# Whole weights loaded and rounded on GpSimd for the third and fourth products, in a fused attention and two-layer kernel

## The reference

```python
scores = scale * np.matmul(q, k.transpose(0, 1, 3, 2))      # 4 batches, 12 heads, 448 tokens, head size 64
scores = cap * np.tanh(scores / cap)
attn = softmax(scores)                                      # the sum plus 1e-09
x = np.matmul(attn, v)                                      # put together to 1792 x 768
gate = 1.0 / (1.0 + np.exp(-(x @ w_gate)))                  # 768 x 1536
z = (gate * (x @ w_val)) @ w_out                            # 1536 x 768
h = z @ w_in                                                # 768 x 2048
y = (h * np.cos(h)) @ w_out2                                # 2048 x 768
```

## Time and profile before

| | us |
|---|---|
| median of 3 runs | 1211.96 (1211.85 to 1212.06) |
| the profiled execution | 1210.31 |
| its span, first to last instruction | 1208.3 |
| TensorE busy | 1197.2 (99%) |
| VectorE, ScalarE, GpSimd busy | 634.4, 558.5, 516.1 |
| moved by DMA | 293.95 MB, of it 58.98 MB written to HBM |

### The profile page before, as it was taken

The page is one execution under the profiler, slowest core; times in us unless marked ns, Lnnn a source line. Parts: engine busy times, 40 slices in busy tenths (PEclk is TensorE's granted clock), DMA queues, the critical chain, the costliest instruction groups (busy, mean ns, idle before and its releaser), DMA issues.

```text
span 1208.3 us, 16807 instructions
## 1 busy us (share of the span) xinstructions
PE 1197.2 (99%) x5932; PEld 1090.2 (90%) x5932; DVE 634.4 (53%) x1227; ACT 558.5 (46%) x1053; POOL 516.1 (43%) x458
## 2 busy tenths in 40 slices
PE   7999999999999999999999999999999999999998
PEld 5779999999999999999999999999999999999998
DVE  8951158876763477776651255877662211105610
ACT  8941155656541467766650257766662011105610
POOL 7969968879653356661113416663302000000000
PEclk9999999999999999999999999999999999999999
DMA  4579986799777678787668668887768566666663
GB/s 160 163 244 324 321 304 232 244 324 322 294 269 253 216 249 247 241 259 263 244 223 278 237 202 269 252 246 243 252 226 265 194 225 211 216 220 217 240 232 108
DMA packets 137746, 293.95 MB, mean 243 GB/s; under 512 B 48192, under 2 KB 57152, under 8 KB 137664
## 3 DMA queue, kind: packets, MB, share of 16 engines
q1 hardware_dynamic: 134064, 287.37, 70.7%
q10 hardware_dynamic: 3600, 5.51, 1.2%
HBM read 219.39 MB, written 58.98 MB: 230 GB/s over the span
## 4 chain that ended last, share of the span: by engine, by line
PE 95%; ACT 2%; DVE 2%; issue 1%; DMA 0%; SPq 0%; ACTq 0%
PE acc L846 27%; PE acc L847 27%; PE acc L845 27%; PE s_ps L743 3%; PE s_ps L744 3%; PE acc L798 2%; PE t_ps L815 2%; PE t_ps L817 1%; PE t_ps L780 1%; PE t_ps L764 1%; PE acc L835 1%; PE acc L837 1%; ACT prob L1030 1%; ACT h_lo_whole L1045 0%; DMA qk_in_whole<-qk 0%
## 5 line engine op out<-in xcount | busy, mean ns | idle before, releaser
L845 PE MATMUL acc<-h_hi,w_hi 128*128 128x448 f32 x672 | 247.8, 369 | 0.0
L846 PE MATMUL acc<-h_lo,w_hi 128*128 128x448 f32 x672 | 246.0, 366 | 0.0
L847 PE MATMUL acc<-h_hi,w_lo 128*128 128x448 f32 x672 | 245.7, 366 | 0.0
L845 PE MATMUL acc<-x_hi,w_hi 128*128 128x448 f32 x576 | 211.3, 367 | 0.0
L846 PE MATMUL acc<-x_lo,w_hi 128*128 128x448 f32 x576 | 210.9, 366 | 0.0
L847 PE MATMUL acc<-x_hi,w_lo 128*128 128x448 f32 x576 | 210.8, 366 | 0.0
L566 POOL TENSOR_TENSOR pt_lo<-pt_lo_whole,pt_hi 128x1344 fp32r<-128x1344 f32 x24 | 75.0, 3126 | 218.5 <-ACT pt_hi L1074 218.5
L847 PE MATMUL acc<-z_hi,w_lo 128*128 128x448 f32 x384 | 140.4, 366 | 0.0
L845 PE MATMUL acc<-z_hi,w_hi 128*128 128x448 f32 x384 | 140.4, 366 | 0.0
L846 PE MATMUL acc<-z_lo,w_hi 128*128 128x448 f32 x384 | 140.4, 366 | 0.0
L847 PEld LDWEIGHTS acc<-h_hi,w_lo 128*128 128x128 f32 x672 | 126.4, 188 | 10.0
(11 more groups left out here) (142 smaller groups left out, 2052.0 us busy)
## 6 DMA issues: line engine op xcount, KB each, us to landing
w_lo<-w_pair SPq DMA_DIRECT2D x156, 384.0 KB, 3.9
w_hi<-w_pair SPq DMA_DIRECT2D x156, 384.0 KB, 3.2
w_lo_whole<-w SPq DMA_DIRECT2D x52, 384.0 KB, 4.0
w_pair<-w_lo SPq DMA_DIRECT2D x52, 384.0 KB, 4.7
w_pair<-w_hi SPq DMA_DIRECT2D x52, 384.0 KB, 5.1
w_lo<-w_pair SPq DMA_DIRECT2D x36, 512.0 KB, 4.3
w_hi<-w_pair SPq DMA_DIRECT2D x36, 512.0 KB, 3.6
qk_in_whole<-qk SPq DMA_DIRECT2D x35, 512.0 KB, 6.2
```

The source lines that it names most:

```text
L845: e.matmul(out[:, 0:S], w_hi[u % HI][:, wb, :], a_hi[:, kb, :], start=first, stop=False)
L846: e.matmul(out[:, 0:S], w_hi[u % HI][:, wb, :], a_lo[:, kb, :], start=False, stop=False)
L847: return e.matmul(out[:, 0:S], w_lo[u % LO][:, wb, :], a_hi[:, kb, :], start=False, stop=last)
```

## The change

The high parts of the third and fourth products' weights are no longer stored. In batches 1 to 3 their whole weights are loaded from the inputs into the w_hi tiles, and GpSimd rounds them where they lie, in an instruction that stands one half ahead in the third product and two ahead in the fourth. TensorE waits for that rounding in place of the load. The waits of the other units are written anew. GpSimd's work for one attention pair in the third product stands at other places.

```diff
+KEPT_UNITS = FIRST[3]
+ROUNDED_AHEAD = {3: 1, 4: 2}
...
-    w_hi = [sb(f"w_hi{p}", [P, 2 * HALF_MAX, P], F32R) for p in range(HI)]
+    w_hi, w_hi_whole = zip(*[sb_both(f"w_hi{p}", [P, 2 * HALF_MAX, P]) for p in range(HI)])
...
-    kept = {s: nc.dram_tensor(f"w{s}_pair", (UNITS_OF[s], 2, 2, P, BLK[s], P), F32, kind="Internal").ap()
+    kept = {s: nc.dram_tensor(f"w{s}_pair", (UNITS_OF[s], 2, 1 + (FIRST[s] < KEPT_UNITS), P, BLK[s], P), F32, kind="Internal").ap()
...
+    def rounded_in_place(b, u, h):
+
+        return 2 * ((b - 1) * (UNITS - KEPT_UNITS) + u - KEPT_UNITS) + h + 1
+
+    def high_loaded(b, u):
+
+        return 16 * ((u + (b - 1) * UNITS) // HI + 1)
...
-                e.dma_start(kept[stage][j, h, 1, :, :, :], f32(w_lo[u % LO])[:, part, :]).then_inc(s_lokept[u % LO][h], 16)
-                e.dma_start(kept[stage][j, h, 0, :, :, :], f32(w_hi[u % HI])[:, part, :]).then_inc(s_hikept[u % HI][h], 16)
+                e.dma_start(kept[stage][j, h, 0, :, :, :], f32(w_lo[u % LO])[:, part, :]).then_inc(s_lokept[u % LO][h], 16)
+                if u < KEPT_UNITS:
+                    e.dma_start(kept[stage][j, h, 1, :, :, :], f32(w_hi[u % HI])[:, part, :]).then_inc(s_hikept[u % HI][h], 16)
...
                 e.wait_ge(s_acc, 2 * (u - HI) + h + 1)
-                e.dma_start(f32(w_hi[u % HI])[:, part, :], kept[stage][j, h, 0, :, :, :]).then_inc(s_hild[u % HI][h], 16)
+                if unit_no(stage, j) < KEPT_UNITS:
+                    e.dma_start(f32(w_hi[u % HI])[:, part, :], kept[stage][j, h, 1, :, :, :]).then_inc(s_hild[u % HI][h], 16)
+                else:
+                    w = {3: w3, 4: w4}[stage]
+                    e.dma_start(w_hi_whole[u % HI][:, part, :], w[j, h, :, :, :]).then_inc(s_hild[u % HI][h], 16)
...
+            def round_w(b, stage, j, h):
+
+                u, part = unit_no(stage, j), slice(h * HALF_MAX, h * HALF_MAX + BLK[stage])
+                e.wait_ge(s_hild[u % HI][h], high_loaded(b, u))
+                rounded(w_hi[u % HI][:, part, :], w_hi_whole[u % HI][:, part, :]).then_inc(s_round, 1)
+
+            def round_ahead(b, n):
+
+                for stage in ROUNDED_AHEAD:
+                    m = n + ROUNDED_AHEAD[stage]
+                    if m < len(halves) and halves[m][0] == stage:
+                        round_w(b, *halves[m])
...
-                if stage == 3 and 2 * j + h in (3, 5):
-                    moved_low(first + FOURTH // NG, j - 1)
-                if stage == 3 and 2 * j + h == 4:
+                if stage == 3 and 2 * j + h in (5, 8):
+                    moved_low(first + FOURTH // NG, (j - 2) // 2)
+                if stage == 3 and 2 * j + h == 6:
                     split_v(first + FOURTH // NG, 1)
...
-                    n, u = u + (b - 1) * UNITS, u + b * UNITS
-                    e.wait_ge(s_hild[u % HI][h], 16 * (n // HI + 1))
-                    e.wait_ge(s_lold[u % LO][h], 16 * (n // LO + 1))
+                    if u < KEPT_UNITS:
+                        e.wait_ge(s_hild[u % HI][h], high_loaded(b, u))
+                    else:
+                        e.wait_ge(s_round, rounded_in_place(b, u, h))
+                    e.wait_ge(s_lold[u % LO][h], 16 * ((u + (b - 1) * UNITS) // LO + 1))
```

More of the change, by code:

```diff
@@ L174, in build @@
     s_wld = [[sem(f"w_whole_loaded{p}{h}") for h in range(2)] for p in range(LO)]
-    s_whi, s_wsplit = sem("w_hi_done"), sem("w_split")
+    s_whi, s_wsplit, s_round = sem("w_hi_done"), sem("w_split"), sem("w_hi_rounded_in_place")
     s_hikept = [[sem(f"w_hi_kept{p}{h}") for h in range(2)] for p in range(HI)]
@@ L381, in unit_no @@
         return FIRST[stage] + j
+    halves = [(stage, j, h) for stage in (1, 2, 3, 4) for j in range(UNITS_OF[stage]) for h in range(2)]
+    def rounded_in_place(b, u, h):
+        return 2 * ((b - 1) * (UNITS - KEPT_UNITS) + u - KEPT_UNITS) + h + 1
+    def high_loaded(b, u):
+        return 16 * ((u + (b - 1) * UNITS) // HI + 1)
     block = nc.Block()
@@ L433, in all_kept @@
                     for p in range(HI):
-                        e.wait_ge(s_hikept[p][h], 16 * len(range(p, UNITS, HI)))
+                        e.wait_ge(s_hikept[p][h], 16 * len(range(p, KEPT_UNITS, HI)))
                     for p in range(LO):
@@ L440, in load_low @@
                 e.wait_ge(s_acc, 2 * (u - LO) + h + 1)
-                e.dma_start(f32(w_lo[u % LO])[:, part, :], kept[stage][j, h, 1, :, :, :]).then_inc(s_lold[u % LO][h], 16)
+                e.dma_start(f32(w_lo[u % LO])[:, part, :], kept[stage][j, h, 0, :, :, :]).then_inc(s_lold[u % LO][h], 16)
             def load_high(b, stage, j, h):
@@ L505, in behind @@
                     move_other_blocks(pair_of(b, i + 1), r // 2)
-            halves = [(stage, j, h) for stage in (1, 2, 3, 4) for j in range(UNITS_OF[stage]) for h in range(2)]
             def just_done(b, n):
@@ L624, in split_w @@
                     e.wait_ge(s_acc, 2 * (u - HI) + h + 1)
-                    e.wait_ge(s_hikept[u % HI][h], 16 * (u // HI))
+                    e.wait_ge(s_hikept[u % HI][h], 16 * (min(u, KEPT_UNITS) // HI))
                 rounded(hi, whole).then_inc(s_whi, 1)
@@ L711, in _ @@
             for b in range(B):
[L712 to L720, removed]
+                for n, (stage, j, h) in enumerate(halves):
+                    if b == 0 and (stage, j, h) not in early:
+                        split_w(stage, j, h)
+                    if b == 0:
+                        split_heads(b, stage, j, h)
+                    if b > 0:
+                        round_ahead(b, n)
+                    if b > 0 and heads_beside(b):
+                        split_beside(b, stage, j, h)
         @block.tensor
```

## The result

The changed kernel takes 1419.77 us (median of 4 runs, 1418.65 to 1420.55) against 1212.01 us (4 runs, 1211.85 to 1212.34) for the one before: a ratio of 1.1713, 95% interval 1.1693 to 1.1733. The profiled execution has a span of 1417.7 us, 209.4 more than before. The prediction was 1420 us, in a range of 1365 to 1460.

A forecast was written before the change was run, and what follows sets the result against it. TensorE, 99% busy, was taken to bound the kernel. Span 1208.3 + 3.7 to the median + stores 0 + rounding 0 + batch 1 13 + batch 2 162 + clock 33 = 1420 us, range 1365 to 1460.

The forecast's parts named there:

- What bounds the kernel: Whole kernel: TensorE, 99% busy, is the limit; what is off it can give back 3.5 us at most.
- Stores: Batch 0: 12.6 MB of stores go, which TensorE did not feel; worth 0.
- Rounding: Batches 1 to 3: 80 us of GpSimd beside TensorE, tightest at half 43; value 0, bound 1.3 us.
- GpSimd's new places: Third product: moved GpSimd work has its reader in the fourth product, over 35 us later; 0.
- The wait for low parts: weights_in picks the wrong low-tile semaphore; 22 halves of batch 2 wait for loads two units ahead: 162 us.
- The clock: Batch 2: TensorE's clock falls to 0.50 for 3.4 us after each wait; 22 x 1.7 = 37, 33 us taken.
- Batch 1: Waits for loads one unit ahead: plain loads make it, those behind block moves don't; 10 to 17 us, value 13.
- That the clock stays up: Rival, batch 2: the waits come but the clock does not fall; 1387 us, chance 0.20.
- Cheap waits: Rival, batch 2: quiet transfers make each wait 4.4 us; 1322, or 1355 us with some clock loss; chance 0.09.
- growing backlog: Rival, batch 2: late moves delay later ones, 22 waits at 11 us are 242; 1500 us with the clock; chance 0.09.
- Relief of HBM: Rival, batch 0: the missing 12.6 MB of stores give back 39 us; 1381 us, chance 0.01.
- not slower: Rival, batches 1 and 2: the wrong semaphore's wait is always met beforehand; 1212 us, chance 0.03.

The follow-up runs named there:

- the run with the stores back: Changed kernel with the right low-tile semaphore, and batch 0's 28 stores of high parts (12.6 MB) put back: 1211.70 us, ratio 0.9997.
- the run with the right index: Changed kernel with one line undone: weights_in again chooses the low tile's semaphore by the running number, (u + 32 b) mod 3: 1210.62 us, ratio 0.9996.
- the quiet run: Changed kernel with the right semaphore, but twenty halves of batch 3 also wait for the low load two units ahead: 1345.32 us, ratio 1.1098.
- the changed order on SyncE: Changed kernel, wrong semaphore kept; SyncE issues the next half's low load right behind the high load, ahead of block moves: 1377.10 us, ratio 1.1367.
- the filled runs: Changed kernel with small unused matmuls ahead of batch 2's 22 waits: 1426.02 us (too long), 1390.70 with fewer; 1337.47 with low loads also issued earlier.
- the second run: Kernel before the change, with only the low tile's semaphore chosen by the batch's own u mod 3, count unchanged: 1417.02 us, ratio 1.1697.
- the rounding twice: Changed kernel with the right low-tile semaphore, and each of the 84 roundings in place done twice: 1214.10 us, ratio 1.0015.
- the one with fewer fills: Changed kernel with 15 to 39 small unused matmuls ahead of each of batch 2's 22 waits: 1390.70 us, ratio 1.1490.

## Why the prediction was right, step by step

- **What bounds the kernel.** Right. TensorE did feel only what made it wait, as the stores (0), the roundings (0) and batch 3 (248.1 before and after) show. That the third product runs "at one pace, whatever the transfers do" was too strong; see the last section.
- **Stores: 0.** Right, by the run with the stores back. The Trainium skill's rule that HBM is almost always the bottleneck (SBUF — State Buffer, "A bandwidth-pool intuition that's wrong") would have given an estimated 39 us here (12.6 MB at 321 GB/s); in this kernel TensorE is the limit and the measurement decides against it.
- **Rounding: 0, bound 1.3.** Right, and the row was near: an instruction in place takes 0.83 us, and in the run with the right index half 43's rounding ends at 572.21 where 572.1 was forecast.
- **GpSimd's new places: 0.** Right in the sum, but the step looked only at who reads the moved work, not at what had stood in the rounding's way. Left where it was, it would have cost 35 us, and the sum would have needed that term.
- **The wait for low parts.** Right in cause and count, and in kinds but for one wait. By the starts of the matmuls and SyncE's rows, ten waits have only the high load ahead of the low one and are 48.6 us (nine and 44 forecast), six stand behind the last moves or a v load, 43.5 us (seven and 56 forecast), six behind eight moves, 55.0 (six and 65): 147 in place of 162. The sizes of the two long kinds came from the earlier trace rows, where the queue was busier. There the moves took 6.35 us and here 5.09. That less is in flight once TensorE stands still would explain it; no run was made for that.
- **The clock.** Right in mechanism, and the price per wait was the term that failed: "22 x 1.7 = 37" and 33 taken, 48.0 measured. The trace has 22 stretches of lower clock in batch 2, one for each wait, but they are not all 3.4 us long. Windows of the changed kernel, a wait of the long kind (idle, then at work), and behind two plain ones:

```profile
748.00:754.50 6.50, 0.00 (x0) 0.00 (x0) 0.00 (x0) 0.00 (x0) 0.00 (x0) 0.50 0.49 130
754.50:758.20 3.70, 3.58 (x10) 3.23 (x11) 0.00 (x0) 0.00 (x0) 0.00 (x0) 0.50 0.00 0
1010.80:1014.20 3.40, 3.10 (x8) 2.81 (x9) 0.86 (x2) 0.29 (x1) 0.15 (x1) 0.50 0.00 0
...
1045.70:1051.70 6.00, 5.93 (x16) 5.31 (x17) 0.20 (x1) 0.00 (x0) 0.00 (x0) 0.50 0.00 0
```

  TensorE works at 0.50, the 1.2 GHz level, for 3.1 to 6 us after a wait. Half of that is lost, 2.2 us on the mean, and the quiet run gives the same 2.2. The earlier trace rows showed one such stretch, and one row was taken for all. The Trainium skill (TensorE: Matmul & The Clock Gate, "HAM oscillation — how this bites in real kernels") tells of a kernel whose clock falls behind the wait for a transfer in every tile, and batch 2 agrees, 22 times of 22. But not every wait does it: the nine of batch 1, of 2.8 us at most, left the granted clock at 1.00.
- **So 1420 was hit by luck, with two errors that cancel:** the waits 18 us too dear (162 against 143.7 idle), the clock 15 too cheap (33 against 48.0). That leaves the sum 3.3 too high. Batch 1 took 2.7 us more than its 13 and batch 0 2.0 that the sum did not have, so it is 1.4 too low; and the median lies 2.1 us over the profiled span where the sum had 3.7, which takes the last 1.6 back.
- **Batch 1.** 13 forecast, 15.7 measured, in nine waits before line 876 (13.1 us); the changed order on SyncE takes 13.6 us of it away. That plain loads one unit ahead are free was shown in batch 3.
- **Rivals.** That the clock stays up would have been 1387; the filled runs put it near there (1390.70), but only by adding work. Cheap waits of 4.4 us hold in batch 3 alone. No growing backlog: the waits behind eight moves stay at 9.0 to 9.6 us through the batch. Relief of HBM fell with the run with the right index, "not slower" with the result.

## What to carry to other kernels

When a wait names a semaphore out of a ring and a target count, both must come from the same running number. With a wrong one the kernel can come to wait for a transfer that has only just been issued, and the trace shows it as like waits at a fixed period (here every third unit of one batch, and none in another where the numbers agree). The slip has a second side, by the counts, that the time does not show: in the units that wait for a load long past, nothing holds TensorE until the low part of their own has landed. Price such a wait as issue plus flight plus what is queued ahead of it, less the work between issue and use, and add the lower clock as a term of its own, read from more than one stretch. Before putting work onto an engine that has time to spare, look for what on it waits for others just ahead of the new instruction.

## What was not expected of the hardware

**TensorE has two paces at the same granted clock.** The first product of batch 0, between its opening and the attention, before the change and after, and batch 3's third product in the kernel before with the wrong index:

```profile
92.00:146.00 54.00, 54.00 (x268) 50.15 (x267) 8.78 (x14) 8.18 (x15) 50.41 (x45) 1.00 0.94 323
...
92.20:146.20 54.00, 54.00 (x263) 49.05 (x262) 8.78 (x14) 8.19 (x15) 50.16 (x44) 1.00 0.94 322
...
1290.00:1344.00 54.00, 54.00 (x264) 49.03 (x263) 31.10 (x53) 30.08 (x55) 0.00 (x0) 1.00 0.64 214
```

268 matmuls or 263 in the same 54 us, with a half of 3.65 or 3.72 us, and the clock column says 1.00 in each. The slower pace costs 1.45 us in batch 0, where the changed kernel, the quiet run, the stores' run and the rounding twice have it, and 4.9 us in batch 3 of the second run and of the one with fewer fills (253.00 against 248.10 in both). The run with the low load first has the same program in batch 0 as the changed kernel and the faster pace there. So 1.4 of the 2.0 us in batch 0 are this, and are no effect of the change. What sets the pace, and what ends it, stays open.

**Two kinds of VectorE instruction are slowed by GpSimd, the others shown aren't.** Groups by form of batches 1 and 2, in the kernel before, with the right index, and with the rounding twice (busy us and mean ns behind the count). They are the scaling of the probabilities, the maximum over them, and the low part of x:

```profile
L1290 DVE TENSOR_SCALAR prob<-prob,recip 128x448 f32<-128x448 f32 x84 | 55.5, 696 | 1.7
L1274 DVE TENSOR_REDUCE rowmax<-prob 128x2 f32<-128x896 f32 x36 | 39.0, 1084 | 61.7 <-ACT prob L1023 61.7
L1364 DVE TENSOR_TENSOR x_lo<-scratch,x_hi 128x448 fp32r<-128x448 f32 x11 | 10.4, 948 | 7.3 <-ACT x_hi L1100 7.3
```

```profile
L1323 DVE TENSOR_SCALAR prob<-prob,recip 128x448 f32<-128x448 f32 x84 | 62.3, 777 | 1.7
```

```profile
L1325 DVE TENSOR_SCALAR prob<-prob,recip 128x448 f32<-128x448 f32 x84 | 70.9, 879 | 1.7
L1399 DVE TENSOR_TENSOR x_lo<-scratch,x_hi 128x448 fp32r<-128x448 f32 x11 | 12.3, 1120 | 7.7 <-ACT x_hi L1135 7.7
```

The scaling goes from 696 to 777 to 879 ns as GpSimd's work grows, and the low part of x, whose two inputs both lie in SBUF, from 948 to 1056 to 1120. The maximum stays: 1084 before, 1082 in the last run. Taken one by one in the kernel before, 52 scalings with no GpSimd instruction beside them take 441 to 456 ns, and 32 with one take 1094 on the mean and 3225 at most; the low part of x takes 625 alone and up to 1666. The Trainium skill (SBUF — State Buffer, "Who interferes with whom") says that a tensor_scalar can take the port pair that VectorE shares with GpSimd and is then held up by it, and that a tensor_reduce can't; the trace agrees. With the right index it cost nothing, as TensorE doesn't wait for VectorE there.
